# A first-tile reorder in a dynamic-convolution and MLP kernel: six PSUM banks, other waits, a third TensorE transpose

## What is computed

```python
w = exp(weight_gen - max(weight_gen, -1)); w = w / (sum(w, -1) + 1e-9)   # (4, 4096, 8, 7)
x_pad = concatenate([zeros((B, 6, 192)), x], axis=1)                      # x: (4, 4096, 192)
conv[b, s, h, :] = sum over k of w[b, s, h, k] * x_pad[b, s + k, h, :]    # 8 heads of 24
h = conv.reshape(16384, 192) @ w_in                                       # w_in: (192, 2048)
g = maximum(0.01 * h, h)
out = g @ w_out                                                           # w_out: (2048, 192)
```

## Time and profile before

| quantity | value |
|---|---|
| three runs | 1062.98, 1063.20, 1065.38 us, median 1063.2 us |
| profiled execution | 1063.15 us |
| its span in the profile | 1061.3 us |
| granted TensorE clock, mean | 0.998 |
| PE busy | 1052.1 us, 99% |
| DVE busy | 770.5 us, 73% |
| ACT busy | 632.5 us, 60% |
| POOL busy | 463.4 us, 44% |

### The profile page before, as it was taken

How to read it: one execution, slowest core, us unless ns; L and a number is a source line. 1 busy time by engine, 2 the same in 40 slices (tenths; PEclk the granted TensorE clock), 3 DMA queues, 4 the chain that set the end, 5 groups by cost and what they waited for, 6 DMA issues and landing times.

```text
span 1061.3 us, 20777 instructions
## 1 busy us (share of the span) xinstructions
PE 1052.1 (99%) x8787; PEld 720.8 (68%) x8787; DVE 770.5 (73%) x1109; ACT 632.5 (60%) x1332; POOL 463.4 (44%) x369
## 2 busy tenths in 40 slices
PE   8999999999999999999999999999999999999998
PEld 3666676676667667667766766766676676677666
DVE  7999867787775877758687677877758777586711
ACT  6766555565556556556655555655565565566554
POOL 0003444455445445435544444554454454455433
PEclk9999999999999999999999999999999999999999
DMA  8101303102121121212203031021321212111010
GB/s 259 48 30 34 94 19 94 33 24 86 33 79 34 39 76 28 79 34 65 63 16 93 19 94 33 23 87 33 79 33 34 82 29 79 33 34 33 16 33 16
DMA packets 67685, 57.03 MB, mean 54 GB/s; under 512 B 56524, under 2 KB 60748, under 8 KB 65608
## 3 DMA queue, kind: packets, MB, share of 16 engines
q1 hardware_dynamic: 67468, 55.41, 18.6%
q10 hardware_dynamic: 124, 0.29, 0.1%
HBM read 29.34 MB, written 12.58 MB: 40 GB/s over the span
## 4 chain that ended last, share of the span: by engine, by line
PE 95%; DVE 3%; SPq 1%; DMA 1%; ACT 0%; issue 0%; POOL 0%; DVEq 0%; ACTq 0%; POOLq 0%
PE out_ps L856 32%; PE out_ps L865 15%; PE h_ps L814 10%; PE h_ps L815 10%; PE h_ps L817 10%; PE h_ps L816 10%; PE h_ps L830 6%; DMA rawD<-in_moe_w_in_dram 1%; DVE gl L582 1%; DVE conv L540 1%; SPq L286 0%; DVE prod L533 0%; SPq L289 0%; DVE wo L562 0%; PE t_ps L856 0%; ACT wo_abs L353 0%
## 5 line engine op out<-in xcount | busy, mean ns | idle before, releaser
L255 POOL TENSOR_TENSOR gl<-g,gh 128x512 f16<-128x512 f32 x360 | 461.3, 1309 | 590.0 <-ACT g L382 590.0
L380 ACT ACTIVATE gh<-h_ps 128x512 f16<-128x512 f32 x512 | 319.1, 623 | 391.4 <-PE h_ps L833 391.4
L856 PEld LDWEIGHTS out_ps<-wo,gh 128*128 128x128 f16 x4064 | 329.0, 98 | 54.2 <-issue 53.4
L856 PE MATMUL out_ps<-wo,gh 128*128 128x192 f16 x4064 | 359.4, 246 | 0.3 <-DVE wo L562 0.3
L582 DVE TENSOR_TENSOR gl<-g,gh 128x512 f16<-128x512 f32 x152 | 132.8, 887 | 269.8 <-ACT g L382 269.8
L382 ACT ACTIVATE g<-h_ps 128x512 f32<-128x512 f32 x512 | 323.7, 632 | 0.0
L540 DVE TENSOR_TENSOR conv<-conv,prod 128x768 f32<-128x768 f32 x186 | 229.6, 1234 | 1.1
L533 DVE TENSOR_TENSOR prod<-xbuf,taps 128x768 f32<-128x768 f32 x186 | 202.7, 1102 | 0.0
L814 PE MATMUL h_ps<-xT,whA 128*128 128x512 f16 x504 | 191.5, 380 | 0.5 <-ACT g L382 0.5
L815 PE MATMUL h_ps<-xT,wlA 128*128 128x512 f16 x504 | 191.5, 380 | 0.0
L817 PE MATMUL h_ps<-xT,whA 128*128 128x512 f16 x504 | 191.5, 380 | 0.0
(11 more groups left out here) (82 smaller groups left out, 410.3 us busy)
## 6 DMA issues: line engine op xcount, KB each, us to landing
xbuf<-in_x_dram SPq DMA_DIRECT2D x15, 1344.0 KB, 5.9
out_dram<-stage SPq DMA_DIRECT2D x31, 384.0 KB, 2.3
taps<-in_weight_gen_dram SPq DMA_DIRECT2D x16, 224.0 KB, 5.9
xT_again<-xT SPq DMA_DIRECT2D x30, 64.0 KB, 2.1
rawO<-in_moe_w_out_dram SPq DMA_DIRECT2D x4, 384.0 KB, 9.9
rawA<-in_moe_w_in_dram SPq DMA_DIRECT2D x2, 512.0 KB, 8.5
xbuf<-in_x_dram SPq DMA_DIRECT2D x2, 384.0 KB, 6.9
rawD<-in_moe_w_in_dram SPq DMA_DIRECT2D x1, 512.0 KB, 7.4
```

Source lines behind the costliest of these rows:

```text
L255: nc.gpsimd.tensor_tensor(gl[:, f % RING, :], g[:, f % RING, :], gh[:, f % RING, :], ALU.subtract).then_inc(s_gl_p, 1)
L380: nc.scalar.activation(gh[:, f % RING, :], h_ps[f % GROUP][:], ACT.Prelu, scale=SHRINK, alpha=SLOPE).then_inc(s_gh, 1)
L856: nc.tensor.matmul(out_of(m, j), gh[:, f % RING, j * P:(j + 1) * P], wo[:, f, part, :], start=f == 0 and (j % 2 == 0 or alone) and part == ...
```

## The change

1. `h_of` lets tile 0's hidden blocks go round six PSUM banks (the four of `h_ps` and the two transpose banks) in place of four.
2. The halo loads no longer wait for a zeroed strip: POOL zeroes the strip of partitions 32, 64 and 96 alone, DVE that of partition 0, the loads write the others, and ACT issues its four loads first of all.
3. The last four softmax instructions of the second half of the first chunk's taps move from before the seven products to behind `take_transposed(0)`; the first two convolution products of tile 1 move together behind two lo pieces.
4. `xT_again` of the PE-transposed tiles is copied by POOL from `xT` in place of ACT from PSUM.
5. `BY_PE` is 3: tile 2 is transposed by PE as well.
6. Step 2's lo products are put off to step 3, behind its hi products (`project_hi`, `project_lo`); DVE waits for them (`s_late_lo`) ahead of its first gl of tile 1. ACT's first `leaky` of tile 1 waits for DVE's gl.
7. In tile 2 DVE's gl block stands at the head of steps 0 and 1.
8. `abs_wo(1)` goes behind the first splits of ACT; the second w_in load of the D rows holds two pieces; `spread_top(1)` goes into `hidden(1)` behind its second block.

```diff
+        t2_32_ps = ps("t2_32_ps", [P, 512])
-        BY_PE = 2
+        BY_PE = 3
+        first_banks = [bank[:] for bank in h_ps] + [t32_ps[:], t2_32_ps[:]]
+        def h_of(m, f):
+            return first_banks[f % len(first_banks)] if m == 0 else h_ps[f % GROUP][:]
...
-            nc.gpsimd.memset(xbuf[:, 0, 0:HALO * D], 0.0).then_inc(s_halo_zero, 1)
+            pool.wait_ge(s_w_sum, 1)
+            for b in range(1, B):
+                p = b * PART_SEQ
+                nc.gpsimd.memset(xbuf[p:p + 1, 0, 0:HALO * D], 0.0).then_inc(s_halo_zero, 1)
+                pool.wait_ge(s_halo_zero, b)
...
+            for t in range(BY_PE):
+                pool.wait_ge(s_xT_a, 2 * (t + 1))
+                nc.gpsimd.tensor_copy(xT_again[DR:P, t % 2, :].rearrange("p (j c) -> p j c", c=P), xT[0:DR, t % 2, :, 1, :]
+                                      ).then_inc(s_xT_p, 1)
...
-            sp.wait_ge(s_halo_zero, 1)
-            load_last_rows(1, 0, PIECE, 1)
+            load_last_rows(1, 0, 2 * PIECE, 1)
-            load_last_rows(1, PIECE, FF, 2)
+            load_last_rows(1, 2 * PIECE, FF, 2)
...
-                if b == 1:
-                    nc.scalar.copy(xT_again[DR:P, t % 2, :], t_ps[0:DR, b, :]).then_inc(s_xT_a, 1)
...
+                    if n == NG:
+                        act.wait_ge(s_gl_v, NF - RING + f + 1)
...
-                if n == 3:
-                    take_transposed(1, 1)
+                if i == NG - 1 and m + 1 < BY_PE:
+                    take_transposed(m + 1, 1)
-                if n == 2:
-                    leaky(3, 0, 2)
-                    take_transposed(1, 0)
-                    leaky(3, 2, GROUP)
+                if i == NG - 2 and m + 1 < BY_PE:
+                    leaky(n + 1, 0, 2)
+                    take_transposed(m + 1, 0)
+                    leaky(n + 1, 2, GROUP)
...
+            for b in range(B // 2, B):
+                load_halos(act, b)
-            act.wait_ge(s_halo_zero, 1)
-            for b in range(B // 2, B):
-                load_halos(act, b)
-            for n in range(2):
-                abs_wo(n)
+            abs_wo(0)
-            for n in range(2, N_PIECES):
+            for n in range(1, N_PIECES):
                 abs_wo(n)
...
+                late = m == 2 and i < 2
+                if late:
+                    lo_of_g(n * GROUP + GROUP - 1, n % NG * GROUP + GROUP - 1)
-                elif n > 2 * NG:
+                elif not late:
...
                 take_transposed(0)
+                for n in range(2, N_SOFTMAX):
+                    softmax0(1, n)
+                lo_pieces(2, 4)
                 dve.wait_ge(s_softmax0[1], N_SOFTMAX)
                 dve.wait_ge(s_chunk[0], DMA)
-                conv1(0, 1)
-                lo_pieces(2, 4)
-                conv1(1, 2)
+                conv1(0, 2)
                 w_top(1)
...
+                dve.wait_ge(s_late_lo, 1)
                 group(NG)
...
-                for n in range(6):
+                convolve(3, 0)
+                take_transposed(2)
+                for n in range(1, 6):
                     convolve(3, n)
...
+                if t == 1:
+                    pe.wait_ge(s_g, NF - 5)
...
-                    if n > 0:
+                    if m > 0:
                         pe.wait_ge(s_g, m * NF + f - GROUP + 1)
+                    elif f >= len(first_banks):
+                        pe.wait_ge(s_g, f - len(first_banks) + 1)
...
+                    if f == GROUP + 1 and m == 0:
+                        spread_top(1)
...
-                project(n)
+                project_hi(n)
+                if i == NG - 2 and m + 1 < BY_PE:
+                    transpose_hi(m + 1)
+                if n == 2:
+                    return
+                if n == 3:
+                    project_lo(2)
+                if n < NG * TILES - 1:
+                    project_lo(n)
+                else:
+                    last_lo()
```

More of the change, by code:

```diff
@@ L157, in dynconv_mlp @@
         s_xT_v = sem("s_xT_v")
+        s_xT_p = sem("s_xT_p")
         s_xT_again = sem("s_xT_again")
@@ L164, in dynconv_mlp @@
         s_gl_p = sem("s_gl_p")
+        s_late_lo = sem("s_late_lo")
         s_out_ps = sem("s_out_ps")
@@ L337, in split_hi @@
                 raw, hi, _ = pieces[piece]
-                if piece[0] == "D" and piece[1] < 2:
-                    act.wait_ge(s_rawD[piece[1] + 1], DMA)
+                if piece[0] == "D" and piece[1] % 2 == 0:
+                    act.wait_ge(s_rawD[piece[1] // 2 + 1], DMA)
                 act.wait_ge(s_w_scale, scales_done(piece))
@@ L371, in take_transposed @@
                 nc.scalar.copy(xT_block(t % 2, b), t_ps[:, b, :].rearrange("p (j c) -> p j c", c=P)).then_inc(s_xT_a, 1)
[L372 to L374 removed]
             def leaky(n, first=0, last=GROUP):
                 for f in range(n % NG * GROUP + first, n % NG * GROUP + last):
+                    h = h_of(n // NG, f)
                     act.wait_ge(s_h, n // NG * NF + f + 1)
[L380 removed]
+                    if n == NG:
+                        act.wait_ge(s_gl_v, NF - RING + f + 1)
+                    nc.scalar.activation(gh[:, f % RING, :], h, ACT.Prelu, scale=SHRINK, alpha=SLOPE
                                          ).then_inc(s_gh, 1)
[L382 removed]
+                    nc.scalar.activation(g[:, f % RING, :], h, ACT.Prelu, scale=SHRINK, alpha=SLOPE
                                          ).then_inc(s_g, 1)
@@ L597, in step @@
                     for k in range(CONV_IN[i]):
-                        if n == 2 * NG and k == 2:
-                            lo_of_g(n * GROUP + GROUP - 1, GROUP - 1)
                         convolve(m + 1, CONV_AHEAD + sum(CONV_IN[b] for b in range(i)) + k)
@@ L727, in _ @@
             nc.vector.memset(junk[:], 0.0).then_inc(s_junk, 1)
+            nc.vector.memset(xbuf[0:1, 0, 0:HALO * D], 0.0).then_inc(s_junk, 1)
             dve.wait_ge(s_taps0, DMA)
-            for ops in (range(0, 2), range(2, N_SOFTMAX)):
-                for half in range(2):
-                    for n in ops:
-                        softmax0(half, n)
+            for half in range(2):
+                for n in range(2):
+                    softmax0(half, n)
+            for n in range(2, N_SOFTMAX):
+                softmax0(0, n)
             dve.wait_ge(s_softmax0[0], N_SOFTMAX)
             dve.wait_ge(s_x0, (1 + 2 * B) * DMA)
+            dve.wait_ge(s_halo_zero, B - 1)
+            dve.wait_ge(s_junk, 2)
             for k in range(K):
@@ L776, in hidden_by_pe @@
                 par = m % 2
-                pe.wait_ge(s_xT_a, 3 * m + 1)
+                pe.wait_ge(s_xT_a, 2 * m + 1)
                 if m == 0:
@@ L843, in wait_lo, with project_hi @@
                     pe.wait_ge(s_gl_p, ((m - EARLY) * NF + f) // GROUP * (GROUP - 1) + f % GROUP + 1)
-            def project(n):
+            def project_hi(n):
                 m, i = n // NG, n % NG
-                fs = range(i * GROUP, (i + 1) * GROUP)
-                for f in fs:
+                for f in range(i * GROUP, (i + 1) * GROUP):
                     pe.wait_ge(s_gh, m * NF + f + 1)
@@ L858, in project, with lo_product, project_lo, last_lo @@
                                              skip_group_check=True)
-                if n == 2:
-                    transpose_hi(1)
-                def lo_products(f, j):
-                    nonlocal ins
-                    ins = nc.tensor.matmul(out_of(m, j), gl[:, f % RING, j * P:(j + 1) * P], wo[:, f, 0, :],
-                                           start=False, stop=f == NF - 1, skip_group_check=True)
-                ins = None
-                if n < NG * TILES - 1:
-                    for f in fs:
-                        wait_lo(m, f)
-                        for j in range(SUB):
-                            lo_products(f, j)
-                            if f == NF - 1 and j % 2 == 1:
-                                ins.then_inc(s_out_ps, 1)
-                else:
-                    for f in fs:
-                        wait_lo(m, f)
-                    for j in range(SUB):
-                        for f in fs:
-                            lo_products(f, j)
-                        if j > 0:
-                            ins.then_inc(s_out_ps, 1)
+            def lo_product(m, f, j):
+                return nc.tensor.matmul(out_of(m, j), gl[:, f % RING, j * P:(j + 1) * P], wo[:, f, 0, :],
+                                        start=False, stop=f == NF - 1, skip_group_check=True)
+            def project_lo(n):
+                m, i = n // NG, n % NG
+                for f in range(i * GROUP, (i + 1) * GROUP):
+                    wait_lo(m, f)
+                    for j in range(SUB):
+                        ins = lo_product(m, f, j)
+                        if f == NF - 1 and j % 2 == 1:
+                            ins.then_inc(s_out_ps, 1)
+                if n == 2:
+                    ins.then_inc(s_late_lo, 1)
+            def last_lo():
```

(13 more changed lines are left out.)

14 lines of the change are left out of this document (6 added, 8 removed).

## The result

| quantity | before | changed |
|---|---|---|
| median of 6 runs each | 1063.24 us | 1071.42 us (1070.03 to 1073.62) |
| profiled execution | 1063.15 us | 1071.83 us |
| its span | 1061.3 us | 1070.0 us |

The ratio is 1.0076, 95% interval 1.0063 to 1.0089: slower by some 8.2 us, outside the range given (1062.6 to 1067.3), where 1065.9 was forecast. No rival of the prediction reaches it by itself either. The busy shares on the page tell nothing of it: PE stands at 99% as it did.

A forecast was written before the change was run, and what follows sets the result against it. PE, without a gap, was taken to bound steps from 91 us (8.057 us each), DVE's chain the start until 49.54. +1.76 up to hidden(4) and +0.96 for tile 2 made +2.72: 1063.15 to 1065.9 us, range 1062.6 to 1067.3.

The forecast's parts named there:

- Halo loads: At the start: the D rows land 0.2 us earlier, bounded by 0.3 later and 1.13 earlier.
- Softmax split: Before the products nothing is won; behind take_transposed(0) DVE's stretch takes 4.55 us for 4.03, so 0.52 later.
- POOL's copy: Behind take_transposed(0): a POOL copy of 0.86 us holds DVE's softmax tensor_scalar by 0.2, bounds nothing and 0.91.
- rival C: Behind take_transposed(0): POOL's copy holds DVE's list by over 0.7 us; at 0.91 the time is 1066.6 us; chance 0.2.
- Six banks, given back: hidden(1) starts about 25.1 us, not 27.33, at full clock; the some 2 us gained are gone by step 2's projection.
- Lo products put off: From step 2's projection to hidden(4): PE stalls 1.7 us on ACT where 0.46 stood, so +1.24.
- Rival B: At hidden_by_pe: ACT's g's are not held up, PE doesn't stall, 1063.8 us; chance 0.14.
- Tile 2 by PE: Around step 6: 12 more transposes 0.68, DMA wait removed 0.08, stall on ACT's g's 0.36; sum +0.96 us.
- Tile 2, DVE's gl first: Head of step 8: DVE idles some 3.4 us for a g, tile 3's transpose goes at 112.7; costs nothing.
- Sum: Whole kernel: 1.76 + 0.96 = +2.72 us on 1063.15, giving 1065.9 us.
- The signs: In the profile after: named moments for w_top(0), w_top(1), hidden(1), step 2's projection, PE's release and later steps of 8.057 us.

The follow-up runs named there:

- ninth experiment: The kernel before, unchanged, run once more for a second profile (one execution): 1063.98 us.
- fourth experiment: The changed kernel with the halo loads as before (waiting for the zeroed strip, ACT's behind its table load): 1070.10 us, ratio 1.0066.
- eleventh experiment: Changed kernel with tile 2, lo products, halo loads, softmax, abs_wo(1), DVE's early order and D loads as before, spread_top(1) behind hidden(1)'s first block: 1063.15 us.
- fifth experiment: The kernel of the second experiment with step 2's lo products back in step 2, ahead of hidden_by_pe(1): 1064.66 us, ratio 1.0014.
- first two experiments: The changed kernel with DVE's take_transposed(2) behind the sixth convolution instruction, 1066.94 us; and with tile 2 by DMA transpose again, without that copy, 1065.94 us.
- third experiment: The changed kernel with POOL's first gl of tile 2 held until DVE has made its last gl of tile 1: 1069.44 us, ratio 1.0058.
- second experiment: The changed kernel with tile 2 by DMA transpose again (BY_PE = 2) and no DVE copy of its third block: 1065.94 us, ratio 1.0027.
- first experiment: The changed kernel with DVE's take_transposed(2) moved behind the sixth convolution instruction, just ahead of step 7's gl: 1066.94 us, ratio 1.0038.
- eighth experiment: The kernel of the second experiment with ACT's halo loads behind its table load in its list, still unwaited: 1065.81 us, ratio 1.0031.

## Why the prediction was wrong, point by point

**Halo loads: wrong in sign, and in what they decide.** The step took "0.2 earlier", bounded by 0.3 later and 1.13 earlier, and asked only when the D rows land. The products start 1.41 later in the profile (1.11 later than in the ninth experiment), and undoing the loads alone gives back 1.3 of the median, of which some 0.7 to 0.8 are the loads' own (fourth experiment). Two things were missed: the halos themselves land later (unwaited, in seven profiles, the products start at 8.66 to 9.08; waited, in seven, at 7.67 to 8.61), and from the products to x_top runs a chain of its own, PE's 7.99 us of sums, which before was level with ACT's sums and left no slack. In both profiles x_top comes 8.48 behind the first product (7.67 to 16.15, 9.08 to 17.56). The text held that "behind them DVE only idles longer"; in the changed kernel what DVE idles for there is PE.

**Softmax split: right in sign, a little dear, and for the wrong reason.** Priced at +0.52 on DVE's list; the list lost 0.35 in the profile. That nothing is won in front is right, but because the halos bound the products (fourth experiment), not because ACT does.

**POOL's copy (rival C): no hold at the place that was named.** There it took 0.61, not 0.86. Timeline of the changed kernel:

```profile
23.41 0.61 POOL L275 COPY xT_again<-xT 64x512 f16<-64x512 f16 x1 [17.89 <-ACT xT L390]
...
23.64 0.37 DVE L498 TENSOR_REDUCE tap_stat<-taps 128x32 f32<-128x224 f32 x1
```

It fell on a one-input reduction that took its usual time (0.38 in the earlier trace rows), and the tensor_scalar behind it took 0.18. In the eleventh experiment the same copy fell on a two-input product, which usually takes 0.95:

```profile
22.33 0.61 POOL L270 COPY xT_again<-xT 64x512 f16<-64x512 f16 x1 [19.47 <-ACT xT L386]
22.56 1.20 DVE L548 TENSOR_TENSOR conv<-xbuf,taps 128x768 f32<-128x768 f32 x1
```

For tile 2 in the changed kernel it took 0.95, and the two products beside it 2.23 in place of 1.82. Rival C's mechanism is real, but a copy's price is 0.25 to 0.41, not 0.7.

**Six banks, given back: held.** `hidden(1)` starts at 26.51, which is the 25.1 of the forecast and the 1.41 of the start, and the clock stays full. `hidden(2)` waits 0.51 and `hidden(3)` 0.86 for DVE's pieces, and PE's projection of step 2 waits 0.45 for DVE's wo.

**Lo products put off: right.** Forecast +1.24, with waits of 0.8, 0.1 and 0.78; the profile has waits of 0.68, 0.38 and 0.47 and +1.3, and the fifth experiment gives 1.28 back. Rival B falls.

**Tile 2 by PE: the step that failed.** The transposes and the stall of PE were right: forecast +0.96, 1.00 in the ladder, 1.0 between the first two experiments. But "DVE's copy of 0.42 and POOL's go into spare time of both" priced the instruction and not the wait in front of it. DVE did have the time; it did not have the order. The copy stands five convolution instructions ahead of the gl, DVE reaches it 5.4 us before PE has made what it takes, and the gl of step 7, not the copy, are what arrives late: +4.6 at step 8. Shown twice: the copy moved behind the convolution (-4.5), and the copy gone (-5.5, of which 1.0 is the transposes). The wait by itself costs little: 0.23 at step 8 with POOL silent. What makes +4.61 of it is where it puts the gl: beside POOL's, 2.89, and behind PE's stalls a half clock, 1.49. The first is shown by an edit (third experiment); the second by two profiles with the same stalls, one with the half clock and one without (fourth experiment), and it was not switched off by an edit of its own. Five of the six executions of the changed kernel have the lower mean clock; the one that hasn't took 1070.03 and lies outside the range too.

**Tile 2, DVE's gl first: nothing, as forecast.** In the second experiment DVE waits 2.68 for that g (3.4 forecast) and the steps around it still take 8.05 to 8.06. In the changed kernel, from 107.85 to the end, every step takes 8.057: (1058.54 - 107.85) / 118 = 8.057.

**Sum.** 1.41 + 0.35 + 1.3 + 1.0 + 4.6 = 8.7, the difference of the spans; the prediction had -0.2, +0.72, +1.24, +0.96 and nothing in the place of these. Without the copy's wait the forecast of 1065.9 would have stood 1.0 under the first experiment, which is the change with that one wait mended; that remainder is about what the halo loads cost more than forecast, less what DVE's list cost less.

**The signs.** Three of those named as right did not come: w_top(0) waited for nothing, at 16.16 (near 15.7 after over 2 us of idle was named), w_top(1) came at 28.02 (26.8) and step 2's projection at 51.35 (50.1). Two came: `hidden(1)` at full clock, and PE released by ACT's g at 56.05 (55.8). The later steps are 8.057 but for 9.14 at tile 2's start, as named (9.1), and for the 12.67 behind it, which was not.

**Open.** Why SP's halo loads, issued 0.2 earlier, land later. Whether it is ACT's lead, which the eighth experiment left almost whole, or SP's own, or that the two queues' first loads overlap in another order, no run here tells apart. Nor is it known why the same stalls are followed by a half clock in some executions and not in others.

## What to carry to other kernels

Idle time of an engine with a list written in order is no price list: for each wait put into it, find the moment at which the list gets there, the moment at which the thing awaited exists, and who waits for what is queued behind; the difference, not the instruction's length, is the cost. Work that becomes late can then run beside an engine that it used to miss (here 2.89 of the 4.61), and a stall of PE can be followed by a stretch at half clock (1.49 of it). Where executions of one kernel differ, compare those with the same granted clock before a difference is put down to the edit. And a load issued earlier is not always a load landed earlier: the halo load of SP's that DVE waits for was issued 0.1 earlier here (2.65 for 2.76) and landed at 9.00, where all of them had landed by 7.67 before.

## What the runs showed of the hardware that was not expected

- **DVE and POOL hold each other in two-input operations.** Four gl of DVE took 5.37 us beside POOL and 2.48 with POOL silent; a convolution instruction 1.87 and 0.95; but a one-input reduction beside POOL's copy was not slower. The Trainium skill (SBUF — State Buffer, SBUF: two separate sides) says that the shared port pair is an exclusive lock, and that of DVE's operations those in a two-port mode or with two SBUF inputs (the latter against a GpSimd operation that reads SBUF) take part in it. These rows agree, and the earlier trace rows have a tensor_scalar of one input held too (1.08 for 0.17).
- **Half clock behind short stalls of PE, in some executions.** In 99 to 101 us PE was busy 0.30 and 0.21 of the time, and the clock was 0.50 from 102 to 104; in the fourth experiment's profile it was busy 0.31 and 0.20 in two such windows, and the clock stayed 1.00. At the start, an idle stretch of 2.79 and one of 2.65 (eighth experiment) were followed by some 3 us of it; 2.17 in the changed kernel's own profile and 2.29 in that of the third were not.
- **Unwaited halo loads take longer, and SP's land later.** Median times from issue to landing, by size (72 and 67.5 KB): SP's 3.2 and 3.5 us before, 5.0 and 5.6 after; ACT's 3.4 and 3.9 before, 3.9 and 4.6 after. Worked out from these, ACT's, issued from 0.73 in place of 1.86, still land some 0.5 earlier, and SP's, issued from 1.67 in place of 1.85, some 1.6 to 1.9 later.
